# A linear-attention scan inside a three-stage kernel: operand preparation of pairs 2 and 3 in pass 0, and a new PSUM bank plan for pass 1

## What is computed

```python
batch, n_heads, seq, head_dim = (2, 8, 768, 48)
for t in range(S):
    cur = np.einsum('bhd,bhe->bhde', u[None] * kt, vt)
    y[:, :, t] = np.einsum('bhd,bhde->bhe', rt, state + cur)
    state = wt[:, :, :, None] * state + np.einsum('bhd,bhe->bhde', kt, vt)
```

## Time and profile before

| | |
|---|---|
| median of 3 runs | 432.8 us (432.79 to 432.83) |
| profiled execution | 433.02 us, of which the traced span is 431.0 us |
| PE busy | 398.7 us, 93% of the span |
| DVE, ACT, POOL busy | 256.0, 169.1, 155.2 us |
| mean granted clock of PE | 0.992 |

### The profile page before, as it was taken

How to read it: one execution, slowest core, us unless ns; L and a number is a source line. 1 busy time by engine, 2 the same in 40 slices (tenths; PEclk the granted TensorE clock), 3 DMA queues, 4 the chain that set the end, 5 groups by cost and what they waited for, 6 DMA issues and landing times.

```text
span 431.0 us, 10442 instructions
## 1 busy us (share of the span) xinstructions
PE 398.7 (93%) x4318; PEld 377.2 (88%) x4318; DVE 256.0 (59%) x515; ACT 169.1 (39%) x349; POOL 155.2 (36%) x173
## 2 busy tenths in 40 slices
PE   2757877999989999989999999999999999999997
PEld 1756867889978899889989999999899999899996
DVE  5969569689443576353534344213798673697662
ACT  4688345576223564223341112112555120555210
POOL 2989331979601653006100116772017010016000
PEclk9999899999998999999999999999999999999999
DMA  8990247654433100000032294540000002000002
GB/s 275 414 410 15 61 164 235 233 152 143 132 138 101 39 2 5 2 2 2 2 122 90 66 396 122 152 135 0 2 0 2 0 2 96 15 0 2 1 20 91
DMA packets 13080, 41.36 MB, mean 96 GB/s; under 512 B 1512, under 2 KB 5610, under 8 KB 12266
## 3 DMA queue, kind: packets, MB, share of 16 engines
q1 hardware_dynamic: 9648, 24.16, 17.1%
q0 software_dynamic: 1008, 13.01, 7.8%
q10 hardware_dynamic: 2378, 3.54, 2.4%
HBM read 37.16 MB, written 4.72 MB: 97 GB/s over the span
## 4 chain that ended last, share of the span: by engine, by line
PE 84%; DVE 4%; POOL 4%; issue 4%; ACT 2%; DMA 1%; SPq 0%; POOLq 0%; DVEq 0%; ACTq 0%
PE PS L1323 24%; PE PS L1325 23%; PE PS L1324 23%; PE PS L1351 5%; PE PS L1407 2%; POOL R L506 2%; POOL WP L491 2%; PE PS L1418 1%; DMA R<-r_dram 1%; DVE ST L995 1%; PE PS L1385 1%; DVE TF L1004 1%; PE PS L1372 1%; PE PS L1514 1%; PE PS L1355 1%
## 5 line engine op out<-in xcount | busy, mean ns | idle before, releaser
L1147 DVE SCALAR_TENSOR_TENSOR HL<-PS,HH 128x384 fp32r<-128x384 f32 x48 | 26.7, 557 | 86.3 <-ACT HH L815 86.2
L815 ACT ACTIVATE HH<-PS 128x384 fp32r<-128x384 f32 x48 | 23.6, 491 | 99.0 <-PE PS L1325 98.8
L1323 PE MATMUL PS<-W2H,HH 128*128 128x384 f32 x144 | 49.8, 346 | 0.0
L1323 PE MATMUL PS<-UTH,W1H 128*128 128x384 f32 x138 | 48.2, 349 | 0.4 <-DVE UTL L1112 0.4
L1325 PE MATMUL PS<-W2H,HL 128*128 128x384 f32 x144 | 48.2, 335 | 0.0
L1324 PE MATMUL PS<-W2L,HH 128*128 128x384 f32 x144 | 48.2, 335 | 0.0
L1325 PE MATMUL PS<-UTH,W1L 128*128 128x384 f32 x138 | 46.7, 339 | 0.0
L1324 PE MATMUL PS<-UTL,W1H 128*128 128x384 f32 x138 | 46.6, 338 | 0.0
L506 POOL TENSOR_TENSOR R<-R,WP 128x384 f32<-128x384 f32 x40 | 39.0, 978 | 12.6 <-ACT UR L680 6.5
L960 DVE TENSOR_TENSOR KW<-KW,WP 128x384 f32<-128x384 f32 x40 | 30.5, 764 | 10.6 <-PE PS L1351 10.1
L1325 PE MATMUL PS<-SGH,ZL 128*128 128x384 f32 x96 | 32.1, 334 | 0.0
(11 more groups left out here) (164 smaller groups left out, 987.8 us busy)
## 6 DMA issues: line engine op xcount, KB each, us to landing
KW<-kw_dram SPq DMA_DIRECT2D x6, 768.0 KB, 6.2
RAW<-w_dram SPq DMA_DIRECT2D x12, 384.0 KB, 4.8
R<-r_dram SPq DMA_DIRECT2D x8, 384.0 KB, 5.5
V<-v_dram SPq DMA_DIRECT2D x8, 288.0 KB, 6.3
W1H<-w_dram POOLq DMA_DIRECT2D x1, 2304.0 KB, 9.6
W2H<-w_dram POOLq DMA_DIRECT2D x1, 2304.0 KB, 9.8
SGH<-w_sgt_dram POOLq DMA_DIRECT2D x1, 2304.0 KB, 11.8
RAW<-w_sgt_dram SPq DMA_DIRECT2D x6, 384.0 KB, 3.3
```

Of the source, the lines that this page charges most:

```text
L815: act.activation(HH[:, f % HSLOT, :], hidden_bank(n, f), ACT.Relu).then_inc(s_hh, 1)
L1147: dve.scalar_tensor_tensor(HL[:, f % HSLOT, :], hidden_bank(n, f), 0.0, HH[:, f % HSLOT, :].bitcast(F32), ALU.max, ALU.subtract).then_inc( ...
L1323: pe.matmul(dst, lh, rh, start=start, stop=False)
```

## The change

**Pass 0.** ACT's `prepare` of pairs 2 and 3 is taken apart. The `UK` copies go to DVE, one each after levels 1, 2, 3 and 4 of pass 0 (`prepare_keys(q, odd)`); the `UR` copies stay on ACT, one each after levels 2, 3, 4 and 5 (`prepare_queries`). The level-0 key updates of pairs 2 and 3 move on DVE from the start of pass 1 into pass 0, behind levels 3 and 4, and have a semaphore of their own, `s_upk0`. The picks of level 0 stay in pass 1.

**Bank plan.** Chunk sums of pairs 0 and 1 both go into banks 4 and 5, except two of pair 1 (k = 8 and 10), which PE writes to bank 6 and ACT copies into `ST[1]` at once. The result of pair 0 goes to banks 6 and 7, at column 96; that of pair 1 to 4 and 5; pair 2 has (0, 2) and (1, 3), pair 3 (6, 7) and (4, 5).

**Order of pass 1.** Transposes and chunk sums of pairs 0 and 1 stand between single scores instead of in couples. `within` of pair 0 is one phase after level 2 and one after level 3, and waits for the first states and the moved sums instead of for all states. `within` of pair 1 leaves pass 1 for the tail, one phase ahead of the chunk sums of pairs 2 and 3 and one behind them; `across` of pair 1 comes behind that. ACT's `store_kt(1)` goes from level 1 to level 2; `first_state(0)` waits for the chunk sums of both pairs. The four idle products ahead of the second stage write bank 7 instead of 5.

The diff's core (the semaphore's declaration, `y_column` in `store_y` and `y_of`, and the order on PE are left out; the latter stands below as rows):

```diff
-            banks = ((4, 5), (6, 7), (4, 5), (0, 2))[q] if q < LANES else (0, 1)
+            banks = ((4, 5), (6, 7), (0, 2), (6, 7))[q] if q < LANES else (0, 1)
...
-            return ((4, 5), (6, 7), (6, 7), (1, 3))[q] if q < LANES else (0, 1)
+            return ((6, 7), (4, 5), (1, 3), (4, 5))[q] if q < LANES else (0, 1)
...
+            bank, at = tail_bank(q, k % 2), k // 2
+            if q == 1:
+                bank, at = tail_bank(0, k % 2), (6, 5)[k % 2] + k // 2
+                if k in MOVED_STATES:
+                    bank, at = tail_bank(1, 0), k // 2 - 4
+            return bank[:, at * HD:(at + 1) * HD]
...
             def first_state(q):
-                act.wait_ge(s_kv, q + 1)
+                act.wait_ge(s_kv, max(q + 1, 2))
+                if q == 1:
+                    first, last = MOVED_STATES
+                    act.copy(ST[q][:, first:last + 1:last - first, :],
+                             tail_bank(1, 0)[:, 0:2 * HD].rearrange("p (k e) -> p k e", e=HD)).then_inc(s_kv_moved, 1)
                 act.copy(ST[q][:, 0, :], kv_of(q, 0)).then_inc(s_s0, 1)
...
                 for q in range(2):
                     right_blocks(q, lev)
-                if lev in (3, 4):
-                    prepare(lev - 1)
+                if lev >= 2:
+                    prepare_queries(2 + (lev - 2) // 2, lev % 2)
...
             for lev in range(NLEV):
                 for q in range(2):
                     keep(q, lev)
+                if 1 <= lev < 5:
+                    prepare_keys(2 + (lev - 1) // 2, (lev - 1) % 2)
+                if lev in (3, 4):
+                    update_k(lev - 1, 0)
             for lev in range(NLEV):
                 for q in range(2, 4):
-                    keep(q, lev)
+                    if lev:
+                        keep(q, lev)
+                    else:
+                        pick(q, 0)
...
             def transpose_k(q):
                 if q == 2:
-                    pe.wait_ge(s_x, 1)
-                if q == 3:
                     pe.wait_ge(s_picked, picks(3, MASKED - 1))
+                if q == 3:
+                    pe.wait_ge(s_x, 1)
...
             def within(q, phase):
                 if phase == 0:
-                    pe.wait_ge(s_moved, 2 * q + 2)
-                    if q == 2:
+                    pe.wait_ge(s_moved, 2 * (3 if q == 2 else q) + 2)
+                    if q == 0:
+                        pe.wait_ge(s_s0, 2)
+                        pe.wait_ge(s_kv_moved, 1)
+                    elif q == 3:
                         pe.wait_ge(s_x, 2)
-                    if q not in (2, 3):
+                    elif q != 2:
                         pe.wait_ge(s_state, states(q, NCH - 2))
```

More of the change, by code:

```diff
@@ L1573, in _ @@
                     score(q, lev)
[L1575 to L1588 removed]
+            score(2, 0)
+            score(3, 0)
+            transpose_k(0)
+            score(2, 1)
+            transpose_k(1)
+            score(3, 1)
+            chunk_states(0)
+            score(2, 2)
+            chunk_states(1)
+            score(3, 2)
+            within(0, 0)
+            score(2, 3)
+            score(3, 3)
+            within(0, 1)
+            score(2, 4)
+            score(3, 4)
+            across(0)
+            score(2, 5)
+            score(3, 5)
             transpose_k(2)
             transpose_k(3)
[L1592 removed]
+            within(1, 0)
             chunk_states(2)
             chunk_states(3)
+            within(1, 1)
+            across(1)
             for q in range(2, 4):
```

95 lines of the change are left out of this document (53 added, 42 removed).

## The result

| | before | the change |
|---|---|---|
| median | 433.37 us (20 runs, 430.86 to 439.98) | 435.32 us (20 runs, 433.49 to 439.91) |
| ratio of the change to before | | 1.0061, 95% interval 1.0037 to 1.0086 |
| profiled execution | 433.02 us, span 431.0 | 439.18 us, span 437.1 |
| mean granted clock of PE in it | 0.992 | 0.973 |

What follows compares the result with a forecast made beforehand. PE's queue in pass 1, then the tail's single thread, was taken as the first stage's bound. States 1.4 and last result copy 1.85 us earlier gave -1.6: 433.02 to 431.4 profiled, median 431.2, range 429.5 to 433.4.

Steps and rivals of the forecast that it cites:

- Price of a new copy on DVE: Pass 0, DVE: each added key copy about 0.5 us, at most 0.66; bounds 0.3 in a gap and 1.65 if stretched.
- The slower rival: DVE becomes late in pass 0; 0.4 us more for each of four moved copies cancels the gain; 434.2 us, chance 0.13.
- DVE at its first level-1 update at 33.1: Start of pass 1: DVE's summed work of pass 0 ends at 33.1 instead of 34.35, 1.2 us earlier.
- First chained states at 38.4: Pass 1, DVE: the chain starts at about 38.4, where it starts before (38.41), so pass 0's 1.2 us are spent.
- The stop of 0.85: Pass 1, PE: a 0.85 us stop, tied to PE's row count, falls in the chunk sums of pair 1, giving 37.9.
- States from 38.4 to 44.4: Pass 1, DVE: same operations as before in this stretch, no change.
- PE's queue before the transposes, 3.9 us shorter: Pass 1 from 44.4, PE: transposes end at 51.1 instead of 55.0, from `within` moved, waits gone and full clock.
- 2.5 us given back on ACT: Tail: first state of pair 3 stands behind pair 1's result copy; 2.5 of 3.9 us lost, states start 1.4 earlier.
- Stop of 1.19 in the chunk sums: Tail, PE: the 1.19 us stop stays in the chunk sums of pairs 2 and 3, which end at 54.8.
- Clock at the upper level from 44 to 50: Pass 1, PE: full clock taken, worth 1.5 us; rival of half clock 432.7 us, chance 0.20.
- The second stage hands the gain on: From 100 us PE is busy 323.64 of 331 us and only shifts; rival that it takes the gain back: 432.8, chance 0.12.
- Size of the effect: Whole kernel: 1.6 us faster, between states 1.4 earlier and last result copy 1.85 earlier; chance of this forecast 0.43.

Runs made afterwards that it cites:

- the probes: Kernel before plus one, or 18, unused VectorE copies, with one or two SBUF inputs; single executions: 432.78 and 433.55 us, then 444.50 and 444.70 us.
- the copies on ACT: The change with the four key copies of pairs 2 and 3 on ACT, level-0 updates still in pass 0: 433.72 us, ratio 0.9971 to before.
- the pause of POOL: The change with POOL waiting for DVE's even key copy of pair 3 before its level-4 decays of pairs 2 and 3: 433.42 us, ratio 0.9971.
- the banks alone: The change's bank plan and order of pass 1, with pass 0 as in the kernel before: 433.94 us, ratio 0.9984 to before.
- the swap: The change with the first state of pair 3 ahead of the result copy of pair 1 on ACT: 436.38 us, ratio 1.0068 to before.
- the column in place of the constant: The change with even key copies of pairs 2 and 3 written as key plus a column of zeros, not times 1: one execution, 437.87 us.
- the load later: The kernel with the copies on ACT, its first-weights high-half load waiting for the second result copy instead of the first: 437.7 us, ratio 1.0091 to before.
- the seven traces of the table: Profiled executions of before, the change and five variants; last result copy at 62.84 to 69.52 us, from there to the end 364.3 to 369.0 us.

## Why the prediction was wrong

- **Price of a new copy on DVE: the step that failed.** I took 0.5 us, "at most 0.66 by the like of pair 0", and kept 1.65 as the far bound (where the prediction says "I take the 0.66 row", its sum still goes by 0.5 to 0.57). Three were 0.41 to 0.75; the fourth took 4.63, outside the bounds. The far bound was the row of an update beside one POOL operation, and I multiplied it by four as if the contest were the same for each. The term that was missing is a wait over several POOL operations in a row, and the row could be read in the trace of before: POOL had no pause from 26.14 to 39.4. Its length is a bound and not a forecast, since the probes beside an unbroken POOL took 0.5 to 1.3; which copy is caught could not have been read from any row. The difference from ratio 1.0061 to 0.9971, some 3.9 us (2 to 6 with both intervals), is this one term, shown by one wait on POOL, which leaves the change as it is, and again by the copies on ACT.
- **The slower rival had the mechanism and the sign**, with 0.13 and 434.2 us. Its place was right (DVE in pass 0, beside POOL), its shape was not: it was to come in small parts from four copies and decided at 0.4 us each; it came as one copy alone. The Trainium skill ("SBUF — State Buffer", section "Who interferes with whom") has a DVE copy with one input, if it runs in a two-port mode, and a GpSimd instruction exclude each other, each for the whole of the other's instruction. The pause that makes 0.35 of 4.63 agrees; a wait from the first of six GpSimd instructions to the end of the last (my expectations, quoted above, say five) is more than that, and here the measurement decides.
- **DVE at its first level-1 update at 33.1**: a second, smaller miss. With the pause of POOL, which takes the long copy out and leaves the others on DVE, it comes at 34.93, 34.1 without the later start: one us late, so of the 1.2 us gained on DVE in pass 0 some 0.2 are left. The last two updates were taken at 1.1 and took 2.31 there. The 33.2 of the copies on ACT is no test of this sum.
- **First chained states at 38.4**: with the copies on ACT 38.6, with the pause of POOL 39.3, both less the start: 0.2 to 0.9 late. The stop of 0.85 that I had put into the chunk sums of pair 1 is there in the first, with 0.59; another of 0.86 stands ahead of a score, where the packet came 0.6 us before PE went on and not 2.4, and is not explained. In the change there is none in the chunk sums. No packet came while PE stood for the long copy (they came at 24.6 and 34.9), so why is open. The copies on ACT:

```profile
32.90 0.92 PE L1405 MATMUL PS<-RM,KW 128*64 128x64 f32 x24 [0.86 <-issue]
...
38.70 0.33 PE L1439 MATMUL PS<-V,KT 64*64 64x48 f32 x7 [0.59 <-issue]
```

- **States from 38.4 to 44.4 "the same operations as before: no change"**: wrong by 0.95. Two states of pair 1 now take the moved sum from SBUF; a link of the chain cost 0.66 to 0.68 there, where the ones from PSUM follow at 0.19. This looks like the same contest: both links end within 0.1 us of the end of a POOL operation beside them (48.49 and 48.43, 49.61 and 49.54), and so they do in the traces of the banks alone (45.83 and 45.76, 46.94 and 46.87) and of the copies on ACT. No run takes POOL away there, so it is not shown.

```profile
47.81 0.68 DVE L1036 SCALAR_TENSOR_TENSOR ST<-ST,WP 128x48 f32<-128x48 f32 x1
48.42 0.60 DVE L1036 SCALAR_TENSOR_TENSOR ST<-ST,WP,PS 128x48 f32<-128x48 f32 x3
48.95 0.66 DVE L1036 SCALAR_TENSOR_TENSOR ST<-ST,WP 128x48 f32<-128x48 f32 x1
```

- **PE's queue before the transposes, 3.9 us shorter**: right in its size, though the parts that the forecast names for it (1.87, 1.17, 1.86 and 1.5) add up to 6.4, since PE also waits for DVE there. From the first update of level 3 to the transposes went 9.1 us before (44.41 to 53.48) and 5.1 in the change (49.52 to 54.64).
- **2.5 us given back on ACT**: the wait is there, 2.65, and the states follow the result copy as reckoned. That it costs was wrong: the swap takes the wait away and gains nothing, since PE is late by its stop.
- **Stop of 1.19 in the chunk sums, "at a count of rows"**: wrong. It left the chunk sums and stood 1.99 in `within` of pair 2. It follows an instruction packet that comes late while the weight load runs. In the sum the tail from the states on took 8.55 us for 5.7. "The loads of the first weights move with it" was the sentence in which I passed over this.
- **Clock at the upper level from 44 to 50**: right for the profiled execution of the change (1.00), but in part luck: it was 0.87 in 40 to 50 with the column in place of the constant and 0.68 with the copies on ACT, and 1.00 again with the load later. In the change the level fell in three other places that I had not named (25 to 35, 63 to 70 and 76 to 80 us).
- **The second stage hands the gain on**: right by the seven traces of the table, apart from the half-clock stretches, which are worth as much.
- **Size of the effect**: the change without the long copy measured 0.9971 in both forms (0.9934 to 1.0008 with the pause, 0.9942 to 1.0001 with the copies on ACT), about 1.3 us less than before, where 1.6 was forecast. The intervals reach from 2.9 us less to no change, so this does not confirm the sum; and that it comes so near is in part luck, since in the trace of the copies on ACT the last result copy is only 0.7 us earlier after the start (54.3 for 55.0), where 1.85 was forecast.

## What to carry to other kernels

Before an operation is moved to VectorE, read GpSimd's row beside its new place: where that row has no pause, a neighbour's duration is only the likely price and the row's length the worst one. Or give GpSimd one wait, which cost 0.76 us here and brought some 3.9. A bulk load is not free because its data is needed late: if TensorE's instructions have to be loaded beside it, TensorE stands, and the trace calls that wait "issue". Cut the load, and try such a cut on the kernel as it is before rebuilding the order around it: here that alone measured 1.1% less.

## What the runs showed of the hardware

- A one-input SBUF copy of VectorE, 128 x 384, took 0.35 us with GpSimd standing and 4.61 to 4.63 us beside a row of GpSimd operations 4.8 us long, in four kernels; in 19 other places, most of them beside GpSimd, 0.34 to 1.66. With two SBUF inputs it took 0.87 in the long place.
- At these stops TensorE goes on 2.2 to 2.9 us after an instruction packet. Beside a weight load of 2.3 MB with the DMA engines some 90% busy, a packet came late and TensorE stood 1.2 to 2.9 us; with the load in two halves the stops were at most 0.6 us. Packets did come during the load in the kernel before (54.7 us) and with the load later (63.4), so the load does not shut them out; the rule behind it is open.
- TensorE's granted clock fell to half in pass 1, with the copies on ACT, after a stretch without any idle time over 1.8 us, and did not fall in another execution of the same code (0.68 and 1.00 in 40 to 50 us). In later stretches too it fell in some traces and not in others with the same code there; each such stretch cost 1.4 to 2.0 us.
